# Routing logits of the first two superblocks as row products on VectorE, spread over the next superblock's steps, in place of transposes and matmuls on TensorE

## What is computed

```python
def _moe2_ref(x, w_gate, w1, w2) -> np.ndarray:
    N, D = x.shape                                  # 2304, 512
    logits = x @ w_gate                             # 8 experts
    expert_idx = np.argmax(logits, axis=1)
    logits_shift = logits - logits.max(-1, keepdims=True)
    probs = np.exp(logits_shift)
    probs /= probs.sum(-1, keepdims=True) + 1e-09
    gate_w = probs[np.arange(N), expert_idx]
    out = np.zeros((N, D), dtype=np.float32)
    for e in range(E):
        mask = expert_idx == e
        xe = x[mask]
        out[mask] = gate_w[mask, None] * (np.maximum(xe @ w1[e], 0.0) @ w2[e])
    return out

def reference(**kwargs):
    attn_out = _attn_ref(**attn_kwargs)             # 4 x 8 x 576 x 64
    x = transposed to 2304 x 512
    x = _moe_ref(x=x, **moe_kwargs)                 # every token through all 8 experts
    return _moe2_ref(x=x, **moe2_kwargs)            # every token through one expert
```

## Time and profile before

| | us |
|---|---|
| median of 3 runs | 1925.79 (1921.24 to 1929.61) |
| the profiled execution | 1926.63, its span 1925.0 |
| TensorE busy | 1900.1 (99%) |
| VectorE busy | 1131.0 (59%) |
| ScalarE busy | 633.8 (33%) |
| GpSimd busy | 1086.3 (56%) |
| a regular step of the first mixture | 15.51 |

### The profile page before, as it was taken

How to read it: one execution, slowest core, us unless ns; L and a number is a source line. 1 busy time by engine, 2 the same in 40 slices (tenths; PEclk the granted TensorE clock), 3 DMA queues, 4 the chain that set the end, 5 groups by cost and what they waited for, 6 DMA issues and landing times.

```text
span 1925.0 us, 32021 instructions
## 1 busy us (share of the span) xinstructions
PE 1900.1 (99%) x11262; PEld 1719.9 (89%) x11262; DVE 1131.0 (59%) x1987; ACT 633.8 (33%) x1107; POOL 1086.3 (56%) x908
## 2 busy tenths in 40 slices
PE   8999999999999999999999999999999999999997
PEld 7889989999998999999999899999999999999997
DVE  4787666566566656555555757555565665322534
ACT  2543343333334333333333433333333332101221
POOL 5766666666587666666667857666666663111111
PEclk9999999999999999999999999999999999999999
DMA  9724444454542222222122222222332223401752
GB/s 229 184 95 148 154 155 152 151 172 159 162 164 69 89 64 78 65 65 65 65 65 66 65 83 88 66 65 65 98 109 95 62 67 115 142 33 57 269 177 71
DMA packets 123356, 209.22 MB, mean 109 GB/s; under 512 B 8910, under 2 KB 58062, under 8 KB 123280
## 3 DMA queue, kind: packets, MB, share of 16 engines
q1 hardware_dynamic: 118240, 192.68, 31.9%
q0 software_dynamic: 5040, 15.51, 2.4%
HBM read 160.03 MB, written 49.19 MB: 109 GB/s over the span
## 4 chain that ended last, share of the span: by engine, by line
PE 95%; DVE 2%; DMA 1%; issue 1%; SPq 0%; ACT 0%; POOL 0%; POOLq 0%; DVEq 0%; ACTq 0%
PE bank L1413 13%; PE bank L1414 13%; PE bank L1415 13%; PE bank L1390 12%; PE bank L1394 12%; PE bank L1392 12%; PE bank L1567 8%; PE bank L1578 2%; PE bank L1577 2%; PE bank L1579 2%; DMA wgraw<-in_moe_w_gate 1%; PE bank L1499 1%; PE bank L1316 1%; PE bank L1347 1%; PE bank L1342 1%
## 5 line engine op out<-in xcount | busy, mean ns | idle before, releaser
L1155 DVE SCALAR_TENSOR_TENSOR acc<-bank,Pw,acc 128x512 f32<-128x512 f32 x516 | 386.5, 751 | 243.4 <-PE bank L1415 231.9
L1415 PE MATMUL bank<-W2H,HL 128*128 128x512 f32 x1152 | 450.3, 391 | 0.0
L1414 PE MATMUL bank<-W2L,HH 128*128 128x512 f32 x1152 | 450.2, 391 | 0.0
L1413 PE MATMUL bank<-W2H,HH 128*128 128x512 f32 x1152 | 450.1, 391 | 0.0
L532 POOL TENSOR_TENSOR W1L<-w1raw,W1H 128x512 fp32r<-128x512 f32 (+1 forms) x190 | 193.8, 1042 | 347.2 <-ACT W1H L692 347.2
L1390 PE MATMUL bank<-XHa,W1H 128*128 128x384 f32 x960 | 323.3, 337 | 2.7 <-ACT Xf L680 0.8
L1394 PE MATMUL bank<-XHa,W1L 128*128 128x384 f32 x960 | 321.1, 335 | 0.0
L1392 PE MATMUL bank<-XLa,W1H 128*128 128x384 f32 x960 | 321.0, 334 | 0.0
L715 ACT ACTIVATE HH<-c 128x384 fp32r<-128x384 f32 x288 | 150.5, 525 | 496.2 <-PE bank L1415 330.2
L1415 PEld LDWEIGHTS bank<-W2H,HL 128*128 128x128 f32 x1152 | 216.2, 188 | 45.3
L1414 PEld LDWEIGHTS bank<-W2L,HH 128*128 128x128 f32 x1152 | 216.3, 188 | 42.5
(11 more groups left out here) (192 smaller groups left out, 2684.2 us busy)
## 6 DMA issues: line engine op xcount, KB each, us to landing
w1raw<-in_moe_w SPq DMA_DIRECT2D x96, 512.0 KB, 3.5
w2raw<-in_moe_w SPq DMA_DIRECT2D x96, 512.0 KB, 3.7
sorted_rows<-blank SPq DMA_DIRECT2D x147, 257.0 KB, 3.6
Wa<-in_moe_w SPq DMA_DIRECT2D x7, 2048.0 KB, 7.9
Wb<-in_moe_w SPq DMA_DIRECT2D x7, 2048.0 KB, 9.3
QK<-qk SPq DMA_DIRECT2D x24, 384.0 KB, 10.3
KV<-kv SPq DMA_DIRECT2D x24, 384.0 KB, 11.7
nxt<-sorted_rows POOLq DMA_DIRECT2D x23, 257.0 KB, 2.9
```

Source lines behind the costliest of these rows:

```text
L1155: ins = nc.vector.scalar_tensor_tensor(tile, psum, weight, tile, ALU.mult, ALU.add)
L1413: mm(dst, HH[:, h, tok], W2H[s][:, m, :], start=(m == 0), stop=False)
L1414: mm(dst, HH[:, h, tok], W2L[s][:, m, :], start=False, stop=False)
L1415: last = mm(dst, HL[:, h, tok], W2H[s][:, m, :], start=False, stop=(m == 1))
```

## The change

Two halves of the work move. The logits of superblocks 0 and 1 (12 tiles) are no longer made on TensorE. ScalarE copies one tile of `acc` into PSUM bank 6 (`tile_copy`), and VectorE multiplies it with each of the 8 gate columns, laid out as whole rows on all partitions, and sums each product along the row (`token_logits`: one instruction for each expert, four in `u2` of one step, four in `u2` of the next). The six tiles of a superblock take the steps 2 to 14 of the next one: j = 2, 4, 6, 9, 11, 13 begin a tile. `choose`, `routing_rank`, `rank` and `place_rows` move from steps 1, 2 and 3 to steps 7, 8, 14 and 15. That is done in step j of the superblock, counted from 0. For this the first four experts of superblocks 1 and 2 are written out, where only the first was, and the loop runs over the fewer that are left. The rows of the gate come from HBM (a new input that holds each gate column 128 times): six stay in `wgr`, and two (`wgr2`) are loaded again for each superblock, since they share memory with other tiles. The loads of the second mixture's first weights move back by one expert (`LEAD_E`).

```diff
+FIRST = (2, 4, 6, 9, 11, 13)
+CHOOSE = (7, 14)
+PEEL = 4
+LEAD_E = E // 2 + 1
...
+            def gate_row_pair(sb):
+
+                sp.wait_ge(s_xh, NP * (sb + 1))
+                sp.wait_ge(s_xl, 5 * (sb + 1))
+                sp.wait_ge(s_xlp, 2 * (sb + 1))
+                sp.dma_start(wgr2[:, :, :], gate_rows[:, 6:8, :]).then_inc(s_wgr2, 16)
+
+            for q in range(NQ):
+                load_ahead(1, 0, q)
+                if q == 0:
+                    gate_row_pair(1)
+                if q < 2:
+                    sp.dma_start(wgr[:, 3 * q:3 * q + 3, :], gate_rows[:, 3 * q:3 * q + 3, :]).then_inc(s_wgr, 16)
...
+            def tile_copy(t):
+
+                act.wait_ge(s_acc, TS * (KS * (t // TS + 1) - 1) + t % TS + 1)
+                if t > 0:
+                    act.wait_ge(s_lgd, 2 * t)
+                nc.scalar.activation(bank[TB][:, :], accs[t // TS][:, t % TS, 0:D], ACT.Copy).then_inc(s_tile, 1)
...
-                if route is not None:
-                    for t in range(TPB):
-                        routing_x(route * TPB + t)
...
                 hidden_hi(k, 0)
+                if tile is not None:
+                    tile_copy(tile)
...
+            def token_logits(t, half):
+
+                dve.wait_ge(s_tile, t + 1)
+                if t + half > 0:
+                    dve.wait_ge(s_lgd, 2 * t + half)
+                if half == 0:
+                    dve.wait_ge(s_wgr, 32)
+                else:
+                    dve.wait_ge(s_wgr2, 16 * (t // TS + 1))
+                for e in range(half * E // 2, (half + 1) * E // 2):
+                    row = wgr[:, e, :] if e < 6 else wgr2[:, e - 6, :]
+                    last = nc.vector.tensor_tensor_reduce(prod[e % 4][:, :], bank[TB][:, :], row, 1.0, 0.0, ALU.mult, ALU.add,
+                                                          lg[:, t, e:e + 1])
+                last.then_inc(s_lgd, 1)
+
             def choose(m):
 
                 ts = slice(m * TPB, (m + 1) * TPB)
-                dve.wait_ge(s_rl, m + 1)
-                l, spread = bank[LGB[m]][:, 0:TPB * E].rearrange("p (t e) -> p t e", t=TPB), [P, TPB, E]
+                l, spread = lg[:, ts, :], [P, TPB, E]
+                if m < NG - 2:
+                    dve.wait_ge(s_lgd, 2 * TPB * (m + 1))
+                else:
+                    dve.wait_ge(s_rl, m - NG + 3)
+                    l = bank[LGB[m]][:, 0:TPB * E].rearrange("p (t e) -> p t e", t=TPB)
...
+                    for half in range(2):
+                        if sb > 0 and j - half in FIRST:
+                            at["u2"] = lambda: token_logits(TS * (sb - 1) + FIRST.index(j - half), half)
+                            break
+                    if sb > 0 and j in CHOOSE:
+                        at["middle"] = lambda: choose(2 * sb - 2 + CHOOSE.index(j))
+                    if sb > 0 and j - 1 in CHOOSE:
+                        at["u2"] = lambda: rank(2 * sb - 2 + CHOOSE.index(j - 1))
...
-                with dve.Fori(3 if sb == 0 else 1, E - 1) as e:
+                with dve.Fori(3 if sb == 0 else PEEL, E - 1) as e:
...
-                    if sb > 0 and q in (1, 2):
-                        pe.wait_ge(s_wg2, 16)
-                        m = 2 * sb - 3 + q
-                        t = m * TPB
-                        after = {1: lambda: routing_T(t), 6: lambda: routing_T(t + 1),
-                                 5: lambda: routing_T(t + 2), 2: lambda: routing_logits(t),
-                                 7: lambda: routing_logits(t + 1), "t0": lambda: routing_logits(t + 2),
-                                 3: lambda: routing_rank(m)}
-                    step(k, q, sb if q == 0 else None, after)
+                    if sb > 0 and j in CHOOSE:
+                        after[3] = lambda: routing_rank(2 * sb - 2 + CHOOSE.index(j))
+                    step(k, q, sb if j == 0 else None, after)
```

More of the change, by code:

```diff
@@ L151, in build @@
         assert a == at_small
+        wgr, _ = place("wgr", [P, 6, D], F32, at_rows + 2 * RSTEP)
+        wgr2, a = place("wgr2", [P, 2, D], F32, at_t + 4 * ND * W)
+        prod = [place(f"prod{i}", [P, D], F32, at)[0] for i, at in enumerate((a, at_t, at_t + 4 * D, at_t + 8 * D))]
+        assert 4 * 6 * D <= RSTEP and a + 4 * D <= at_h
         GH, _ = place("GH", [P, ND, W], F32R, at_x + 3 * 4 * NK * W)
@@ L444, in _ @@
                 load_ahead(1, E - 1, q)
-            with sp.Fori(0, E // 2) as e:
+            for q in range(NQ):
+                load_ahead(2, 0, q)
+                if q == 0:
+                    gate_row_pair(2)
+            with sp.Fori(1, LEAD_E) as e:
                 for q in range(NQ):
@@ L464, in _ @@
             first = sp.value_load(order[0:1, 0:1], min_val=0, max_val=E - 1)
-            for e in (E // 2, E // 2 + 1):
+            for e in (LEAD_E, LEAD_E + 1):
                 for q in range(NQ):
@@ L473, in _ @@
             row1 = sp.value_load(lead_row[0:1, 1:2], min_val=P, max_val=(E - 1) * N + P)
-            for e in range(E // 2 + 2, E):
+            for e in range(LEAD_E + 2, E):
                 for q in range(NQ):
@@ L607, in _ @@
             for sb in range(SB):
-                for q in range(NQ):
-                    step(step_no(sb, 0, q), q)
-                    if sb > 0 and q == 2:
+                for j in range(NQ if sb == 0 else PEEL * NQ):
+                    step(step_no(sb, j // NQ, j % NQ), j % NQ)
+                    if sb > 0 and j == CHOOSE[0] + 1:
                         if sb == 1:
@@ L614, in _ @@
                         place_rows(2 * sb - 2)
-                    if sb > 0 and q == 3:
+                    if sb > 0 and j == CHOOSE[1] + 1:
                         place_rows(2 * sb - 1)
@@ L622, in _ @@
                     nc.gpsimd.dma_start(nxt[:, :], sorted_rows[bass.ds(row0, P), :]).then_inc(s_xs, 16)
-                with pool.Fori(1, E - 1) as e:
+                with pool.Fori(1 if sb == 0 else PEEL, E - 1) as e:
                     for q in range(NQ):
@@ L778, in _, with step @@
                     x_hi(0, 4)
-            def step(k, q, first=False, last=False, sb=0, route=None, late_x=None, scale=None):
+            def step(k, q, first=False, last=False, sb=0, route=None, late_x=None, scale=None, tile=None):
                 if not first:
@@ L824, in _ @@
             for sb in range(SB):
[L825 to L828, removed]
+                for j in range(NQ if sb == 0 else PEEL * NQ):
+                    k = step_no(sb, j // NQ, j % NQ)
+                    step(k, j % NQ, first=(k == 0),
+                         route=2 * sb - 2 + CHOOSE.index(j) if sb > 0 and j in CHOOSE else None,
+                         tile=TS * (sb - 1) + FIRST.index(j + 1) if sb > 0 and j + 1 in FIRST else None,
+                         late_x=sb if j == 0 else None)
                 if sb == 0:
@@ L832, in _ @@
                             step(step_no(sb, e, q), q, scale=(None, grow, part, None)[q] if e == 2 else None)
-                with act.Fori(3 if sb == 0 else 1, E - 1) as e:
+                with act.Fori(3 if sb == 0 else PEEL, E - 1) as e:
                     for q in range(NQ):
@@ L1192, in _ @@
             for sb in range(SB):
-                for q in range(NQ):
+                for j in range(NQ if sb == 0 else PEEL * NQ):
                     at = {}
-                    k = step_no(sb, 0, q)
-                    if q == 0:
+                    e, q = j // NQ, j % NQ
+                    k = step_no(sb, e, q)
+                    if j == 0:
                         at["start"], at["u2"] = (lambda: x_lo(sb, 5, s_xl)), (lambda: x_lo(sb, 6, s_xl))
@@ L1201, in _ @@
                         at["u2"] = lambda: sink_rows(q - 1)
-                    if sb > 0 and q in (1, 2):
[L1203 to L1206, removed]
+                    for half in range(2):
[6 more added lines that the diff above has]
+                        at["u2"] = lambda: rank(2 * sb - 2 + CHOOSE.index(j - 1))
+                    if sb == SB - 1 and j == CHOOSE[1] + 1:
                         at["middle"], at["close"] = (lambda: pick_lead(0)), (lambda: pick_lead(1))
-                    step(sb, k, 0, q, **at)
-                    if q == 0:
+                    step(sb, k, e, q, **at)
+                    if j == 0:
                         if sb == 0:
@@ L1529, in _ @@
             for sb in range(SB):
-                for q in range(NQ):
-                    k = step_no(sb, 0, q)
+                for j in range(NQ if sb == 0 else PEEL * NQ):
+                    q = j % NQ
+                    k = step_no(sb, j // NQ, q)
                     after = {}
@@ L1637 @@
     arrays["attn_tab"], arrays["keep_tab"] = tables()
+    arrays["gate_rows"] = _np.ascontiguousarray(_np.tile(inputs["moe2_w_gate"].T[None], (P, 1, 1)))
     args = [nc.dram_tensor(n, a.shape, _mybir.dt.from_np(a.dtype), kind="ExternalInput").ap()
```

23 lines of the change are left out of this document (12 added, 11 removed).

## The result

The changed kernel takes 1906.47 us (median of 4 runs, 1903.33 to 1910.97), the kernel before 1923.51 beside it (4 runs). The ratio is 0.9902 with a 95% interval of 0.9881 to 0.9923. A second set of runs (6 of the changed kernel, 23 of before) gives 1906.95 against 1924.99 and 0.9913, 0.9890 to 0.9935. These ratios are the measured ones as recorded; they are not the quotients of the two medians, which would be 0.9911 and 0.9906. The profiled execution took 1910.97 us, 15.66 less than that of before; the sum had said 15.7.

A forecast was written before the change was run, and what follows sets the result against it. TensorE, busy for 99% of the span, was taken as the bound. 1926.63 less 16.1 for removed work plus 0.4 for choice steps gave 1910.9, 1910.1 by the median; 1910.5 us was taken, range 1905.5 to 1917.5.

The forecast's parts named there:

- the sum: Whole kernel: 1926.63 - 16.1 + 0.4 = 1910.9 us for an execution like the profiled one.
- The gain: TensorE's queue: transposes and logits of 12 tiles leave, 1.34 us a tile, 16.1 us in all.
- the 0.4 allowed for the choice steps: Steps 7 and 14 of the superblocks: 0.1 us for each of four, as choose may wait for GpSimd.
- The price of a product: VectorE between c12 and c22: 0.70 us a row product plus 0.08 for its read, 3.1 us for four.
- Rival C: Row products on VectorE need two passes: 24 us back (1934.5), or 12 with overlapping reads (1922.5); chance 0.06, half for either.
- The room: VectorE from c12 through c22 to the first gather: 4.7 us before TensorE waits at output tile 3.
- D: Row products between c12 and c22 wait 1 us each for GpSimd's port: 58 us lost, 1968; chance 0.04.
- The products ahead don't lengthen this chain: Choice steps, VectorE's work up to c21: row products add no delay, since the third gather sets it again.
- Rival B: Choice steps: choose waits for GpSimd's sums, c21 up to 1 us late in four steps, 1914.5; chance 0.10.
- rival E: SyncE's load queue: gate rows delay weights beyond 7.46 us of slack, about 6 us once, 1916.5; chance 0.04.
- the one from the profiled execution to the median: Whole kernel: the profiled execution lies 0.84 us above the median, so 1910.9 becomes 1910.1; 1910.5 taken.

The follow-up runs named there:

- the run with eight: Changed kernel with each group of four row products made twice, a semaphore wait between the groups; first mixture 1493.02 us against 1475.77.
- the run with twelve products: Changed kernel with each group of four row products made three times; first mixture 1581.63 us against 1475.77.
- the run from SBUF: Changed kernel with row products reading the acc tile in SBUF, not ScalarE's PSUM copy, which is still made; first mixture 1600.52 us against 1475.77.

## Why the prediction was right, and where not

**The gain.** Right in mechanism and size: 16.1 us were worked out for the work that leaves TensorE, and putting it back costs 16.16. The forecast for an execution like the profiled one, 1910.9, met 1910.97, but that it did so to 0.1 us is luck twice over. The two profiled executions happened to reach the mixture at the same time, 102.20 and 102.27 us, where others of these kernels reach it up to 9 us earlier; and the 0.4 allowed for the choice steps, which wasn't lost there, happened to be the size of the scatter in the unchanged steps.

**The price of a product.** I took 0.70 + 0.08 and it is 0.61 + 0: four take 2.5 us, not 3.1. The mistake was to add the read, which runs beside the next product, and to price the product by its duration (0.685) and not by the distance between starts. The estimate by the Trainium skill's figures ("Vector Engine (DVE) Microarchitecture Reference", section 5.2) had given 0.61 for the product, and the trace agrees, with starts 0.61 us apart; the 0.08 estimated for the read is its row's duration, but not a cost. Rival C, two passes, fell.

**The room.** 4.7 us is confirmed between 3.8 and 5.0, and by the lateness of the run with eight. That a delay within it is handed on to nobody held. What I said of rivals C and D beyond it was too cheap: a missed bank costs 0.2 us more than the lateness, and a wait of 2.8 us costs 1.6 more wherever the clock falls behind it. D with its 2.4 us over the budget would have been, as an estimate from the run with twelve products, some 4 us a step and near 100 us in all instead of 58, if the clock had fallen there too. D's 1 us of waiting, "like the cast", was also a low reading of the earlier trace rows: that cast took 2.33 us where the reduction of the same three results took 0.18. In the run from SBUF a product waited 1.4 us on average, up to 2.2.

**The choice steps.** I allowed 0.1 us each, and they lost nothing beyond the rank product's 0.45 and, in step 78, 0.2 more: forecast at about 15.96, it took 16.18, as said above. VectorE waited for product 4's end before `c21` again, by 0.16 us in step 39:

```profile
719.19 0.56 DVE L1183 TENSOR_TENSOR c<-cs,bank 128x384 f32<-128x384 f32 x1 [0.16 <-PE bank L1454]
```

"The products ahead don't lengthen this chain, since it is set again at the third gather" holds for four and six products, not for eight. Rival B didn't happen.

**The loads.** Nothing was seen of the gate rows on TensorE (rival E): steps 33 and 34 last 15.54 us and step 35 lasts 15.51.

**The range.** The step that failed is the one from the profiled execution to the median, with the allowance "a median can lie some 2 us off". The medians, 1906.47 and 1906.95, lie 4 us under the 1910.5, at the low end of the range, and the first ratio times the median then measured for before (1923.51) gives 1904.7, below it. I had moved from the profiled execution to the median by 0.84 us, as if an execution's distance from its kernel's median were the same for both kernels. It isn't: the profiled execution of the changed kernel was the slowest of its four, 1910.97 among 1903.33 to 1910.97, and lay 4.5 us above their median. The runs show scatter in that term's place: the start of the kernel differs by 10 us between executions, and each kernel is measured with its own draws of it. The second profiled execution of the changed kernel reached the mixture 8.8 us earlier than the first and took 8.2 us less, 1902.73. That the same holds for the executions without a profile, and so for the medians, is likely but not shown. The runs of before already spread over 8 us for three, which should have widened the range by some 3 us on each side, and the part of the work that it comes from, by the two profiles of the changed kernel (the first 96 us), was in the profile to be looked at. That the changed kernel gains more than the 15.7 of the rows isn't shown: both intervals of the ratio hold 0.9919.

## What to carry to other kernels

Where one engine is full, price what leaves its queue by the distances between starts around it, and expect just that. For what another engine takes over, work out the room of the very gap: from when the engine is free, through each operation behind, to when the full engine wants the result; 2.5 us were free in one gap and cost 23 us of the mixture in another on an engine that idles for 37% of the time. And give work for VectorE beside a busy GpSimd one input in PSUM, even for the price of a copy on an idle ScalarE.

## What I had not expected of the hardware

- With a wait of 2.8 us in each of 24 steps TensorE's granted clock fell to 0.50 in 19 of them, mostly for 3.4 us and in step 38 about 1 us after it had begun to work again, and stayed at 1.00 in the other five; beside waits of 0.2 us it stayed at 1.00. An overrun of a gap is therefore not priced by its length alone.
- The read of a row product's sum (0.08 us) costs nothing beside the next product, which starts at the same time.
- The first 50 us, in which the DMA engines are 96 to 98% busy, moved 276 GB/s in one execution and 241 in another of the same kernel, and the mixture began at 93.4 or 102.3 us.
